# Scores of batch 0 for two heads at a time, with the weight preparation divided anew among the engines

## The reference

```python
# attention: 8 heads of 64, causal window of 128, ALiBi bias
scores = (q @ k.T) / 8 + slopes[h] * -abs(i - j)        # only 0 <= i - j < 128
attn   = softmax(scores);  x = attn @ v                 # [B, 576, 512]
# first MLP, with layer norm and a residual
xn = (x - mean) / sqrt(var + 1e-6) * g_ln
x  = x + relu(xn @ w_ch1) @ w_ch2                       # 512 -> 2048 -> 512
# second MLP, gated by a convolution over the sequence (3 taps)
h  = relu(x @ w_in)                                     # 512 -> 1024
out = (h * sigmoid(conv3(h))) @ w_out                   # 1024 -> 512
```

## Time and profile before

| | us |
|---|---|
| median of 3 runs | 798.57 (797.63 to 798.58) |
| the profiled execution, its own time | 799.17 |
| its span | 797.4 |
| PE busy | 782.7, 98% |
| DVE busy | 511.5, 64% |
| ACT busy | 371.5, 47% |
| POOL busy | 172.5, 22% |
| granted TensorE clock | 1.0 of full speed in every slice |

### The profile page before, as it was taken

One profiled execution on the slowest core, in us unless ns is written; L12 is line 12 of the kernel. 1 busy time (PEld: TensorE's weight loads), 2 busy tenths in 40 slices (PEclk: granted clock), 3 DMA queues, 4 the chain that ended last, 5 costly groups with the idle time before them and its releaser, 6 DMA issues.

```text
span 797.4 us, 17024 instructions
## 1 busy us (share of the span) xinstructions
PE 782.7 (98%) x5809; PEld 753.8 (95%) x5809; DVE 511.5 (64%) x1419; ACT 371.5 (47%) x1033; POOL 172.5 (22%) x166
## 2 busy tenths in 40 slices
PE   9989999999999999999999999999999999999998
PEld 6679889999999999989999999999998999999998
DVE  5775778764677776456776645222259888778862
ACT  7783576551355564125565422123244444444432
POOL 6676572110111211011121100111110111011100
PEclk9999999999999999999999999999999999999999
DMA  7763521301312130131213012303220211222001
GB/s 185 185 178 104 162 75 38 105 8 61 105 31 76 45 99 9 61 108 31 76 38 105 9 61 89 114 1 102 88 90 12 87 41 65 82 82 82 22 23 46
DMA packets 56494, 59.42 MB, mean 75 GB/s; under 512 B 25184, under 2 KB 43616, under 8 KB 55904
## 3 DMA queue, kind: packets, MB, share of 16 engines
q1 hardware_dynamic: 56416, 58.43, 24.2%
HBM read 44.25 MB, written 14.16 MB: 73 GB/s over the span
## 4 chain that ended last, share of the span: by engine, by line
PE 75%; issue 11%; DVE 7%; ACT 3%; POOL 3%; POOLq 0%; ACTq 0%; DVEq 0%
PE bank L1383 21%; PE bank L1385 20%; PE bank L1384 20%; PE bank L1322 3%; PE bank L1354 3%; PE bank L1336 2%; PE bank L1281 2%; PE bank L1307 2%; DVE prob L1034 1%; ACT prob L810 1%; PE bank L1294 1%; POOL small L689 1%; PE bank L1270 1%; POOL k_lo L679 1%; DVE q_st L1121 1%
## 5 line engine op out<-in xcount | busy, mean ns | idle before, releaser
L1383 PE MATMUL bank<-xn_hi,wa_hi 128*128 128x288 f32 x512 | 156.1, 305 | 1.4 <-issue 1.4
L1383 PE MATMUL bank<-h_hi,wb_hi 128*128 128x288 f32 x512 | 156.1, 305 | 0.5 <-DVE ch_stage L1102 0.5
L1384 PE MATMUL bank<-xn_lo,wa_hi 128*128 128x288 f32 x512 | 151.7, 296 | 0.0
L1385 PE MATMUL bank<-xn_hi,wa_lo 128*128 128x288 f32 x512 | 151.6, 296 | 0.0
L1384 PE MATMUL bank<-h_lo,wb_hi 128*128 128x288 f32 x512 | 150.8, 295 | 0.0
L1385 PE MATMUL bank<-h_hi,wb_lo 128*128 128x288 f32 x512 | 150.6, 294 | 0.0
L840 ACT ACTIVATE h_hi<-bank 128x288 fp32r<-128x288 f32 x128 | 52.4, 409 | 175.3 <-PE bank L1385 174.2
L1091 DVE SCALAR_TENSOR_TENSOR h_lo<-bank,h_hi 128x288 fp32r<-128x288 f32 x128 | 58.2, 455 | 112.6 <-ACT h_hi L840 110.9
L1383 PEld LDWEIGHTS bank<-xn_hi,wa_hi 128*128 128x128 f32 x512 | 96.5, 188 | 2.9 <-issue 2.0
L1383 PEld LDWEIGHTS bank<-h_hi,wb_hi 128*128 128x128 f32 x512 | 96.3, 188 | 2.5 <-issue 1.2
L1384 PEld LDWEIGHTS bank<-xn_lo,wa_hi 128*128 128x128 f32 x512 | 96.6, 189 | 0.0
(11 more groups left out here) (133 smaller groups left out, 1671.3 us busy)
## 6 DMA issues: line engine op xcount, KB each, us to landing
k_raw<-qkT SPq DMA_DIRECT2D x48, 144.0 KB, 2.8
q_raw<-qkT SPq DMA_DIRECT2D x48, 144.0 KB, 2.9
x_in<-x_spill SPq DMA_DIRECT2D x8, 580.0 KB, 4.1
ch_in<-ch_spill SPq DMA_DIRECT2D x8, 580.0 KB, 5.1
x_spill<-xT SPq DMA_DIRECT2D x4, 1152.0 KB, 4.2
ch_spill<-ch_stage SPq DMA_DIRECT2D x32, 144.0 KB, 1.9
out<-out_stage SPq DMA_DIRECT2D x32, 144.0 KB, 1.8
wa_raw<-w SPq DMA_DIRECT2D x16, 256.0 KB, 3.5
```

The source lines that it names most:

```text
L1383: nc.tensor.matmul(dst, w_h, a_h, start=start, stop=False)
L1384: nc.tensor.matmul(dst, w_h, a_l, start=False, stop=False)
L1385: last = nc.tensor.matmul(dst, w_l, a_h, start=False, stop=stop)
```

## The change

Six edits, all in batch 0's attention and in the weights.

1. **Two heads per score matmul.** `half_qk` becomes two buffers of `[P, 3, 384]`. The even head of a pair lies in partitions 0 to 63 (q in part 0, k in part 1), the odd head in 64 to 127 (q in part 0, k in part 2), the other quarters are zero. One matmul with the two q's stacked as weights' rows and parts 1 and 2 as moving data gives both heads' scores side by side in one bank. All tiles of a pair stand in the even head's slot; the odd head's slot has none. A bank is free once the odd head's minimum is taken.
2. **Bookkeeping that follows.** A new item `HX` keeps the other engines' delays per head. The loads of a pair are issued together, after the last tile of the pair two before. All of c = 1's copies of transposed tiles go to ACT. POOL's clearing of the pads waits for the last `HO`.
3. **Warm matmuls** ahead of the first `HP`: five, not ten.
4. **`w_ch1`'s layout and gain.** A tile is now rows 128d.. and columns 512j.. of the plain matrix, so that the gain is one number per partition and is applied as the scale of ACT's `w_hi`; `w_gain` is gone. DVE makes the low part (a `SCALAR_TENSOR_TENSOR`). Step f of the product needs the four tiles 4(f//4) to 4(f//4)+3. POOL makes both parts of `w_ch2`.
5. **When.** The prologue prepares 6 tiles of `w_ch1` (slots 2.1 to 7.1, one in each) and 12 of `w_ch2`; `first` prepares 10 and 4, the last of them at group 16.45.
6. **The second MLP's weights** come at groups 38.5 to 61 instead of 33 to 63, in another order (`LATE_TILES`), the last four into `wb_lo`.

```diff
-HALF_PROLOGUE = {("HS", 0): -0.3, ("HS", 1): -0.28, ("HP", 0): 1.8, ("HO", 0): 2.75}
+HALF_PROLOGUE = {("HX", 0): -0.3, ("HP", 0): 1.8, ("HO", 0): 2.75}
+PAIR_SCORES = (-0.3, -0.29, -0.28)
...
-WARM = [(1.79, 10)]
+WARM = [(1.79, 5)]
...
-W_TIMES = [2.4, 3.6, 4.8, 6.0, 7.2, 8.4, 9.2, 10.0, 10.8, 11.6, 12.4, 13.2, 14.0, 14.8]
-W_HI_POOL = (4, 8, 12)
-W_PACE, W_AHEAD = 1.5, 6
+W1_PROLOGUE, W1_FIRST = [2.1, 3.1, 4.1, 5.1, 6.1, 7.1], [0.25, 2.05, 3.85, 5.65, 7.45, 9.25, 11.05, 12.85, 14.65, 16.45]
+W2_PROLOGUE, W2_FIRST = [3.0, 4.0, 5.0, 6.0, 7.0, 8.0, 9.2, 10.15, 11.1, 12.05, 13.0, 13.95], [-0.6, 0.6, 1.6, 16.2]
...
 def half_items(c, start, slots, at, heads):
+    pairs = [(start + slots * h + (PAIR_SCORES[x] if c or h else PAIR_SCORES[0] + 0.01 * x), ("HS", c, h, x))
+             for h in heads if h % 2 == 0 for x in range(HNT[c])]
+    return pairs + [(start + slots * h + t, (kind, c, h, x)) for h in heads for (kind, x), t in at.items()]
...
 def copied_by_act(c, h):
-            return c == 1 and 1 <= h <= 5
+            return c == 1
...
+        def hi_by_pool(n):
+            return n < NW1 and not first_layer(n)
+        def lo_by_pool(n):
+            return not first_layer(n) if n < NW1 else n % 2 == 1
...
-                    sp.wait_ge(bank_filled, use_of(0, ("HS", c4, h4, len(HGROUPS[c4]) - 1)) + 1)
+                    for x in range(HNT[c4]):
+                        sp.wait_ge(bank_filled, use_of(0, ("HS", c4, h4 - h4 % 2, x)) + 1)
...
-            def w_gain(n):
-                nc.gpsimd.tensor_tensor(kc, kc, g_col[:].unsqueeze(2).broadcast_to((P, DC, P)), ALU.mult).then_inc(w_prep, 1)
...
-                nc.scalar.activation(w_tile(n)[1], w_raw(n), ACT.Copy).then_inc(w_hi_ready, 1)
+                nc.scalar.activation(w_tile(n)[1], w_raw(n), ACT.Copy, scale=gain(n) if first_layer(n) else 1.0).then_inc(w_hi_ready, 1)
...
+                if first_layer(n):
+                    nc.vector.scalar_tensor_tensor(lo, w_raw(n), gain(n), hi.bitcast(F32), ALU.mult, ALU.subtract).then_inc(w_split_dve, 1)
...
-            for i in range(4):
-                nc.vector.memset(half_qk[i][D:P, :, :], 0.0).then_inc(half_rows_clear, 1)
+            for i in range(2):
+                nc.vector.memset(half_qk[i][D:P, 1, :], 0.0).then_inc(half_rows_clear, 1)
+                nc.vector.memset(half_qk[i][0:D, 2, :], 0.0).then_inc(half_rows_clear, 1)
...
 def half_scores(c, h, x):
-                pe.wait_ge(half_qk_loaded[e % 4], 16 * (e // 4 + 1))
-                for t, at in HGROUPS[c][x]:
-                    rows, q0, k0, keys, _, _ = HTILES[c][t]
-                    last = nc.tensor.matmul(dst[0:rows, at:at + keys], half_qk[e % 4][:, 0, q0:q0 + rows],
-                                            half_qk[e % 4][:, 1, k0:k0 + keys], start=True, stop=True)
+                qk = half_qk[e // 2 % 2]
+                for i in (e, e + 1):
+                    pe.wait_ge(half_qk_loaded[i % 4], 16 * (i // 4 + 1))
+                rows, q0, k0, keys, _, _ = HTILES[c][x]
+                nc.tensor.matmul(dst[0:rows, 0:2 * keys].rearrange("p (h k) -> p h k", h=2), qk[:, 0, q0:q0 + rows],
+                                 qk[:, 1:3, k0:k0 + keys], start=True, stop=True).then_inc(bank_filled, 1)
...
-        out += [(2 * (F1 + m) + 1, ("W", NW1 + m)) for m in range(NW2)]
+        out += [(38.5 + 1.5 * i, ("W", NW1 + i)) for i in range(NW2)]
```

More of the change, by code:

```diff
@@ L126, in half_items @@
 def half_items(c, start, slots, at, heads):
-    return [(start + slots * h + t, (kind, c, h, x)) for h in heads for (kind, x), t in at.items()
-            if kind != "HS" or x < len(HGROUPS[c])]
+    pairs = [(start + slots * h + (PAIR_SCORES[x] if c or h else PAIR_SCORES[0] + 0.01 * x), ("HS", c, h, x))
+             for h in heads if h % 2 == 0 for x in range(HNT[c])]
+    return pairs + [(start + slots * h + t, (kind, c, h, x)) for h in heads for (kind, x), t in at.items()]
 def norm_items(start, c, times=NORM_TIMES):
@@ L137, with last_step @@
 NORM_ORDER = [x[0::2] for _, x in sorted(norm_items(0, 0))]
+LATE_TILES = [0, 1, 12, 2, 3, 13, 4, 5, 14, 6, 7, 15, 8, 9, 10, 11]
+IN_WA = 12
+assert sorted(LATE_TILES) == list(range(NW2))
+def last_step(m):
+    return m // DC * DC + DC - 1
 def is_int(batch):
@@ L166, in timeline @@
         out += [(t, ("WARM", n)) for t, n in WARM]
-        out += [(t, ("W", n)) for n, t in enumerate(W_TIMES)]
+        out += [(t, ("W", n)) for n, (first, t, _) in enumerate(W_TIMES) if not first]
         return sorted(out, key=lambda x: x[0])
@@ L170, in timeline @@
     if kind == "first":
-        out += [(0.25 + W_PACE * (n - W_PROLOGUE), ("W", n)) for n in range(W_PROLOGUE, NW1)]
+        out += [(t, ("W", n)) for n, (first, t, _) in enumerate(W_TIMES) if first]
         out += HALF_FIRST
@@ L297, in build @@
         half_pt0 = sb("half_pt0", [P, 512], scope=half)
-        half_qk2 = sb("half_qk2", [P, 2, 384], scope=half)
+        half_v = [sb(f"half_v{i}", [P, 3, D], scope=half) for i in range(4)]
         half_pt1 = sb("half_pt1", [P, 512], scope=half)
-        half_qk3 = sb("half_qk3", [P, 2, 384], scope=half)
+        sb("half_gap0", [P, 4 * 3 * D], scope=half)
         sb("half_gap1", [P, 2 * S + NT * D], scope=half)
@@ L304, in build @@
         sb("half_gap2", [P, PCOLS + DC * S + 2 * P + 3 * P + SMALL + DC * CH + DC * CH], scope=half)
-        half_qk, half_v = [], []
+        half_qk = []
         for i in range(2):
-            half_qk.append(sb(f"half_qk{i}", [P, 2, 384], scope=half))
-            half_v += [sb(f"half_v{2 * i + k}", [P, 3, D], scope=half) for k in range(2)]
+            half_qk.append(sb(f"half_qk{i}", [P, 3, 384], scope=half))
             if i == 0:
@@ L777, in v_hi, with half_exps @@
                 nc.scalar.activation(v_st[:, :, 0:D], v_raw[:], ACT.Copy).then_inc(v_hi_ready, 1)
-            def half_exps(c, h, x):
-                for t, _ in HGROUPS[c][x]:
+            def half_exps(c, h):
+                for t in range(HNT[c]):
                     rows, _, _, keys, _, col = HTILES[c][t]
@@ L893, in run @@
                         evacuate(batch, a[0])
-                    elif name == "w" and a[0] not in W_HI_POOL:
+                    elif name == "w" and not hi_by_pool(a[0]):
                         w_hi(*a)
@@ L974, in half_minima @@
                 dve.nop(nofuse=True)
-                for t, at in HGROUPS[c][x]:
+                for t in range(HNT[c]):
                     rows, _, _, keys, b0, col = HTILES[c][t]
                     r = half_rows(c, h) + t
+                    item = ("HS", c, h - h % 2, t)
+                    src = bank[bank_of(0, item)][0:rows, keys * (h % 2):keys * (h % 2) + keys]
+                    dve.wait_ge(bank_filled, use_of(0, item) + 1)
+                    dve.nop(nofuse=True)
                     ins = nc.vector.tensor_tensor_reduce(
-                        out=half_prob_of(c, h)[0:rows, col:col + keys], in0=src[0:rows, at:at + keys],
+                        out=half_prob_of(c, h)[0:rows, col:col + keys], in0=src,
                         in1=half_dist[0:rows, h, b0:b0 + keys], scale=-SCALE, scalar=BIG, op0=ALU.add, op1=ALU.min,
@@ L1157, in run @@
                         evacuate(batch, a[0])
-                    elif name == "w" and not by_pool(a[0]):
+                    elif name == "w" and not lo_by_pool(a[0]):
                         w_lo(*a)
@@ L1476, in result @@
                 last = product(out_bank[d % 2][:, 0:CH],
-                               [(wa_hi[:, F2 + f, P * d:P * (d + 1)], wa_lo[:, F2 + f, P * d:P * (d + 1)], g_hi[:, c, f, :],
-                                 g_lo[:, c, f, :], f == 0, f == F2 - 1) for f in range(half * part, half * (part + 1))])
+                               [(*w_out_part(f, d), g_hi[:, c, f, :], g_lo[:, c, f, :], f == 0, f == F2 - 1)
+                                for f in range(half * part, half * (part + 1))])
                 if part == 1:
@@ L1515 @@
         "g_ln": np.ascontiguousarray(inputs["moe_g_ln"].reshape(DC, P).T),
[L1516 removed]
+        "w1": np.ascontiguousarray(inputs["moe_w_ch1"]),
         "w2": np.ascontiguousarray(inputs["moe_w_ch2"]),
```

152 lines of the change are left out of this document (77 added, 75 removed).

## The result

The changed kernel takes 806.93 us (median of 4 executions, 805.57 to 810.31) against 798.52: ratio 1.0113, 95% interval 1.01 to 1.0127. **It is 8.4 us slower**; 796.0 was forecast and 800.0 was the upper end. Its granted clock is 0.998, those of the other three 0.996, 0.994 and 0.998, where the profile of before has 1.0.

A forecast was written before the change was run, and what follows sets the result against it. PE, busy for 98% of the span, was taken as the bound. Prologue -0.85 us and `first` -1.86 us gave -2.7 us: 796.5 against the execution's 799.17, 795.9 against the median, said as 796.0; range 793.3 to 800.0.

The forecast's parts named there:

- The steady loops have the same lists as before and are left out.: Steady loops after `first`: instruction lists unchanged, so no cost or gain was counted there.
- `first`, -1.86 us: PE's idle pieces in `first` shrink with POOL nearly empty of weights: -0.56 - 0.8 - 0.5 us.
- each of ten sticks out by 0.15: Upper bound for `first`: DVE's ten new low parts each delay by 0.15 us and nothing is gained, +1.5 us.
- the gain stops at the prologue: Rival: in `first` DVE becomes late where POOL was and the idle pieces stay; 797.7 us, chance 0.23.
- The start, -0.15 us: Up to the next scores after HO(0): fewer warm matmuls against a 1 us load wait and a bare copy, -0.15 us.
- Scores, -1.8 us: Prologue: paired scores halve the weight loads, saving 0.51 us per c = 0 pair and 0.2 per c = 1 pair.
- The bare copies, +2.7 us: Prologue, h = 2, 4, 6 of c = 0: PE idles 0.9 us each for DVE's now uncovered copy before the outputs.
- DVE just keeps up: Prologue, c = 0 pairs: DVE needs 5.9 us of the new 6.93 us period, which leaves it 1 us.
- The prologue's end, -2.1 us: Idle pieces of 1.30 and 0.62 us and 0.2 of the small rest vanish with POOL's multiplications and ACT's late weights gone.
- +0.5: Prologue, c = 1: part of two copies sticks out although an `IN` or `OUT` stands between, +0.5 us.
- DVE locked out by POOL in the prologue: Rival, slots 2.4 to 7.5: DVE's low parts wait for POOL's, 4.8 us in all, 800.8 us; chance 0.17.
- Edit 6, zero: 460 to 600 us: PE is busy throughout beside the weight preparation, so moving it was costed at nothing.

The follow-up runs named there:

- e1: The changed kernel with eight more already fulfilled waits on PE ahead of its first matmul, nothing else: 803.48 us, ratio 1.0066.
- e4: The kernel before with 165 more PE waits ahead of its first matmul, putting the steady loop's head last in a 16 KB code piece: 821.01 us.
- e9: The changed kernel with one already fulfilled wait on PE ahead of its first matmul: 804.61 us, ratio 1.0079.
- e15: The kernel before with 157 fulfilled PE waits ahead of its first matmul, leaving nine instructions of the code piece from the loop's head on: 818.64 us.
- e2: The kernel before with only the new division of the weights (edits 4 to 6), no pairing: 799.08 us, ratio 1.0006.
- e8: e2 with the ten `w_ch1` weights of `first` spread over groups 0.25 to 8.35 instead of 0.25 to 16.45: 797.58 us, ratio 0.9989.
- e10: e2 with the ten `w_ch1` weights of `first` at groups -0.3 to 2.1 and 6.6 to 9.0: 794.40 us, ratio 0.9944.
- e6: e1 with an odd head's probability transposes moved ahead of the even head's outputs (c = 0): 803.62 us, one execution.
- e3: The kernel before with only the pairing (edits 1 to 3) and eight more PE waits: 805.17 us, ratio 1.0083.
- e14: The kernel before with only the pairing, the first four heads' q/k loads issued first and one PE wait: 803.92 us, ratio 1.0062.
- e11: e9 with the first four heads' q/k loads issued first and e8's weight times: 799.70 us, ratio 1.0011.
- e13: e9 with the first four heads' q/k loads issued first and e10's weight times: 797.47 us, ratio 0.999.

## Why the prediction was wrong

**"The steady loops have the same lists as before and are left out."** This is the step that failed most: 3.3 us of idle time at the jump, and 0.6 us in each pass, that of the second with a slow stretch in it, together 4.6 of the 6.4 us, in a place where no list had changed. That the instructions are the same does not fix where they stand in PE's code (e1, e4, e9 and e15 show it), nor which instruction of POOL lies beside which of DVE (e2 shows it). Not one of the rivals held it, so the range did not either.

**`first`, -1.86 us.** Measured +0.40. The mechanism was named ("two instructions of DVE stood still beside POOL's"), but turned into a gain, since POOL had become "nearly empty". It still had its k and v splits and four weights, and the ten new two-input instructions of DVE were spread over just the groups in which these run. The bound of +1.5 for "each of ten sticks out by 0.15" was nearer; in fact two stuck out, by 0.65 and 1.20 us. The rival "the gain stops at the prologue" is this case, and `first` took 0.4 us more than it said. e8 and e10 show that the mechanism, placed otherwise, would have given the gain forecast, and more: -1.9 and -4.0 us in `first`.

**The start, -0.15 us.** HO(0) came at 14.56 instead of 14.0. The wait for the fourth load was 2.48 us instead of 1, mostly since the first pair took 2.25 us at the full clock, not 3.2 at the lower one: it ended at 6.93, not 8.1, and the load's landing set the time anyway (forecast 9.1, matmul at 9.42). The next scores start at 16.48 instead of 16.04: +0.4.

**Scores, -1.8 us.** A pair of c = 0 takes 2.28 us to the next group (16.48 to 18.76), so 0.36 saved, not 0.51. The first two pairs of c = 1 take 1.82 us each, against 1.93 and 1.82 for the same heads before, the other two 1.72 and 1.74, against 2 x 0.87: 0.11 saved at most, not 0.2. Together some -0.9. The fit through two points gave the record a price that it does not have at 512 columns.

**The bare copies, +2.7 us.** Right: 3 x 0.88 = 2.64, and one in the start. "DVE just keeps up" was right too, but ACT does not: e6 shows its normalising as the next bound, 0.3 to 1.5 us behind. So the one other order that was tried did not win the copies back.

**The prologue's end, -2.1 us.** The piece of 1.30 us shrank to 0.36, the one of 0.62 went, but three others came (0.48, 0.44, 0.25 us), in all 1.53 instead of 2.36 us. e2, without pairs, has two there, 0.23 and 0.18 us: what is left over belongs to the pairs. The forecast had +0.5 for that. The DMA engines were busy for 0.79 of the time from 12.1 to 29.1 us, not nine tenths.

**The rival "DVE locked out by POOL in the prologue"** did not come: the six new low parts there take 0.73 to 1.00 us.

**Edit 6, zero.** Right for `last`, where the preparation lies: the same matmuls stay 6.83 us apart from 481.5 to 606.33 us (times of the kernel before). In the second MLP, from its wait for ACT (1.64 us before, 1.62 after) to the last matmul, it is 188.3 us before and 187.9 after; every kernel with edits 4 to 6 has these -0.4 us, e3 and e14 do not.

With -0.9 + 2.64 - 0.83 + 0.4 the prologue comes to +1.3 of the measured +1.85. A part of the rest is that a wait also takes away the overlap of PE's records: from the transposes at 19.97 to the outputs at 21.66 it is 1.69 us, 0.95 more than the 0.74 without a wait, and not 0.88. The remainder was not followed further.

## What to carry to other kernels

When an edit changes how many instructions stand ahead of a loop, the loop's jump can change by 3 us and cost the clock as well; look at PE's idle time with no releaser at the first pass back, and shift the code by an instruction before judging the edit. A weight's preparation on DVE is free where POOL has nothing beside it or where nobody waits for the next DVE instruction: where to put it was worth 4.7 us, more than which engine makes it. Lists that no edit touched can still meet in another way, and 0.25 us decided over 0.9 (e2 in the steady loop): compare the starts of the same instruction in both traces, stage by stage, before a gain or a loss is put down to the stage where the edit was. And when a cover is taken from a copy, look at the engine after the copy: the order could be mended, but ACT was already due.

## What was not expected of the hardware

At the jump PE resumed 2.2 to 3.0 us after a fetch of 16 KB of its own code began, and the next piece's fetch came 3.1 to 3.8 us after the first (342.78 and 346.17 us in the kernel after, 356.37 and 359.45 in e15), over all kept traces. Behind an idle time of 4.5 us there the granted clock was 0.50 from 349.4 to 352.8 us in the kernel after, and in e4, within and behind its 4.2 us, from 361.1 to 367.9. Idle times of 1.2 to 1.7 us at the same place had no such stretch behind them in any kept trace; in e15 the two of 1.45 and 1.98 us, with four matmuls between them, had one, from 362.9 to 366.3 us. The length of an idle piece does not decide alone: 1.89 us at 50.02 in e3 was followed by one, 1.90 us at the same group in e14 was not. Why one execution of the kernel after takes 805.57 and another 810.31 us, at clocks of 0.998 and 0.994, stays open: the long ones have no trace. e9, e11 and e13 have such executions too, up to 807.53, 805.17 and 801.51 us at 0.993, 0.994 and 0.996.
